# Attention, gated MLP and routed experts on one core: TensorE's operands moved to multiples of 512 bytes

## The reference, cut to what matters

```python
def reference(...):
    # 1. attention: B, H, S, D = 4, 8, 576, 64; each query sees itself and the 63 keys before it
    scores = np.matmul(q, k.transpose(0, 1, 3, 2)) / 8, masked to the window
    x = softmax(scores) @ v, laid out as 2304 tokens x 512
    # 2. gated MLP, d_ff = 1536
    xn = x / np.sqrt(np.mean(x * x) + 1e-06) * rms_g
    g, val = xn @ w_gate, xn @ w_val
    x = (g * sigmoid(g) * val) @ w_out
    # 3. 8 experts, top 2 of noisy logits per token
    noisy = x @ w_gate2 + log1p(exp(x @ w_noise)) * noise
    for e in range(8): out[mask] += weight * (np.maximum(x[mask] @ w1[e], 0) @ w2[e])   # 512 -> 1024 -> 512
```

## The kernel before, in words

| operand | offset | phase |
|---|---|---|
| `w_sb`, `ew_sb` (`W_OFF`) | 16512 | 128 |
| `ident`; `y_sb`, `yT_sb` | 180352; 172160, 166016 | 128 |
| `ones`, `tri`; `onesb` | 181376, 180864; 181120 | 128; 384 |
| `qbd`, `k_sb`, `v_sb`, `p_sb`, `pT_sb` | from 187616 | 224 |
| `mask_sb`, `identb` | 186336, 187360 | 480 |
| `xp`, `hp`, `sq` | 186336, 213984, 220128 | 480 |
| `x_row`, `xTh`, `xTl`, `relu`, `hTh`, `hTl` | from 194528 | 480 |

## Time and profile before

### The profile page before, as it was taken

The page is one execution under the profiler, slowest core; times in us unless marked ns, Lnnn a source line. Parts: engine busy times, 40 slices in busy tenths (PEclk is TensorE's granted clock), DMA queues, the critical chain, the costliest instruction groups (busy, mean ns, idle before and its releaser), DMA issues.

```text
span 1135.4 us, 20144 instructions
## 1 busy us (share of the span) xinstructions
PE 1112.4 (98%) x6285; PEld 961.4 (85%) x6286; DVE 540.7 (48%) x1166; ACT 324.2 (29%) x712; POOL 398.9 (35%) x370
## 2 busy tenths in 40 slices
PE   8999999999999999999999999999999999999996
PEld 7878999999998999999987888888888888888884
DVE  6776344353343443353456744445444544454442
ACT  7995122432331431432451020110202020200231
POOL 3567982022021120200386042240607060421485
PEclk9999999999999999999999999999999999999999
DMA  7975527013031030100356142241515151311565
GB/s 216 275 244 190 167 77 248 1 58 110 1 125 45 19 131 1 56 1 1 131 185 223 48 129 102 82 149 41 190 39 192 46 166 65 116 59 49 179 219 182
DMA packets 82732, 129.39 MB, mean 114 GB/s; under 512 B 6593, under 2 KB 38737, under 8 KB 82673
## 3 DMA queue, kind: packets, MB, share of 16 engines
q1 hardware_dynamic: 60816, 71.20, 19.4%
q10 hardware_dynamic: 16032, 38.47, 10.2%
q0 software_dynamic: 5824, 18.95, 5.1%
HBM read 85.87 MB, written 42.73 MB: 113 GB/s over the span
## 4 chain that ended last, share of the span: by engine, by line
PE 88%; POOL 4%; issue 3%; ACT 2%; DMA 2%; DVE 1%; POOLq 0%; ACTq 0%; DVEq 0%; SPq 0%
PE bank L774 26%; PE bank L965 18%; PE bank L937 18%; PE bank L806 13%; PE bank L978 3%; PE bank L720 3%; PE bank L747 2%; PE bank L949 1%; POOL token_rows_a L661 1%; PE bank L730 1%; PE bank L714 1%; DMA token_rows_b<-expert_rows,slots_u 1%; POOL expert_parts L645 1%; POOL token_rows_a L674 1%; PE bank L842 1%
## 5 line engine op out<-in xcount | busy, mean ns | idle before, releaser
L774 PE MATMUL bank<-x_parts,mlp_weights 128*128 128x384 f32 x1704 | 316.1, 341 | 0.0
L774 PEld LDWEIGHTS bank<-x_parts,mlp_weights 128*128 128x128 f32 x1704 | 300.6, 188 | 5.7 <-issue 0.3
L965 PE MATMUL bank<-expert_parts,hT_high 128*128 (+1 forms) x688 | 220.3, 401 | 1.4 <-DVE hT_low L1647 1.4
L937 PE MATMUL bank<-expert_parts,xT_high 128*128 (+1 forms) x688 | 220.3, 401 | 0.5 <-DVE xT_low L1636 0.5
L645 POOL TENSOR_TENSOR expert_parts<-raw_expert_a,expert_parts 128x512 fp32r<-128x512 f32 x64 | 81.5, 1311 | 266.7 <-ACT expert_parts L1249 266.7
L806 PE MATMUL bank<-mlp_weights,hidden_parts 128*128 128x512 f32 x648 | 163.9, 397 | 1.5 <-ACT y_sb L1173 1.5
L965 PEld LDWEIGHTS bank<-expert_parts,hT_high 128*128 128x128 f32 x688 | 126.3, 188 | 29.1 <-issue 1.7
L937 PEld LDWEIGHTS bank<-expert_parts,xT_high 128*128 128x128 f32 x688 | 126.2, 188 | 28.1 <-DVE xT_low L1636 0.8
L806 PEld LDWEIGHTS bank<-mlp_weights,hidden_parts 128*128 128x128 f32 x648 | 120.5, 188 | 26.2 <-ACT y_sb L1173 1.8
L965 PE MATMUL bank<-expert_parts,hT_low 128*128 (+1 forms) x344 | 136.1, 396 | 0.0
L937 PE MATMUL bank<-expert_parts,xT_low 128*128 (+1 forms) x344 | 136.0, 395 | 0.0
(11 more groups left out here) (205 smaller groups left out, 1244.6 us busy)
## 6 DMA issues: line engine op xcount, KB each, us to landing
raw_expert_a<-in_w ACTq DMA_DIRECT2D x32, 512.0 KB, 3.6
raw_expert_b<-in_w ACTq DMA_DIRECT2D x32, 512.0 KB, 4.0
x_row<-routed_rows SPq DMA_DIRECT2D x43, 256.0 KB, 2.7
expert_rows<-y_row SPq DMA_DIRECT2D x43, 256.0 KB, 2.0
expert_rows<-zeros SPq DMA_DIRECT2D x4, 2304.0 KB, 13.1
v_sb<-in_v SPq DMA_DIRECT2D x32, 256.0 KB, 3.7
q_sb<-in_qT SPq DMA_DIRECT2D x16, 288.0 KB, 3.7
k_sb<-in_kT SPq DMA_DIRECT2D x16, 288.0 KB, 4.2
```

The source lines that it names most:

```text
L774: last = nc.tensor.matmul(bank[:, 0:CHUNK], w_sb[:, i, wp, at:at + P], xp[:, par, part, k, :], start=n == 0, stop=n == 3 * KB - 1)
L937: last = nc.tensor.matmul(ps[half][:, 0:512], (xTh, xTl)[xp][:, k, :], ew_sb[:, bass.ds(slot, 1), wp, k * F2 + half * 512:k * F2 + half * ...
L965: last = nc.tensor.matmul(ps[5][:, 0:D], (hTh, hTl)[hp][:, f, :], ew_sb[:, bass.ds(slot, 1), 2 + wp, f * D:(f + 1) * D].rearrange("p a n - ...
```

## The change

It moves buffers and touches nothing else: every instruction, wait and transfer stays. `W_OFF` goes up by 384 bytes to 16896 (phase 0), and with it the staging area and `WORK_OFF`. `noise_sb`, `route_const` and `tri` leave `keep` for the free bytes behind `logitsT` in the staging area (offsets 179200 to 180608). `ones` now follows `ident` and `onesb` follows `ones`. `identb` moves from before `qbd` to behind `pT_sb` (220672), and `keep` is rounded up to a multiple of 512 (185344), where `att`, `mlp` and `moe` begin. By the code all operands of the table above then have phase 0 (`tri` 128; windows that step by 256 bytes have 0 or 256), and so have `raw_exp_a` and `raw_exp_b`. `rw_sb`, `lg_sb` and the small routing tables have other phases than 0 before and after.

```diff
--- before.py
+++ after.py
@@ -54,8 +54,10 @@
     xs_dram = nc.dram_tensor("routed_rows", [E * STRIDE, D], F32).ap()
     ye_dram = nc.dram_tensor("expert_rows", [ETILES * P, D], F32).ap()
 
+
+    ROW = 512
     base = 16512
-    W_OFF = base
+    W_OFF = (base + ROW - 1) // ROW * ROW
     STAGE_OFF = W_OFF + 6 * 6144 * 4
     WORK_OFF = STAGE_OFF + 4 * 4096
 
@@ -91,18 +93,22 @@
     assert D * 4 + CHUNK_TILES * KB * P * 4 <= 2 * 4096
     lgT_sb = at("logitsT", [P, P], F32, STAGE_OFF + 2 * 4096 + CHUNK_TILES * D * 4)
 
+
+    late = Area(STAGE_OFF + 2 * 4096 + CHUNK_TILES * D * 4 + P * 4)
+    noise_sb = late.take("noise_sb", [P, TILES, E], F32)
+    rc = late.take("route_const", [P, c_route.shape[1]], F32)
+    tri = late.take("tri", [P, P], BF16, 2)
+    assert late.pos <= WORK_OFF
+
     keep = Area(WORK_OFF)
     ident = keep.take("ident", [P, P], F32)
-    tri = keep.take("tri", [P, P], BF16, 2)
+    ones = keep.take("ones", [P, P], F32)
     onesb = keep.take("onesb", [P, P], BF16, 2)
-    ones = keep.take("ones", [P, P], F32)
     g_sb = keep.take("g_sb", [P, KB], F32)
 
     LOGITS = 32
     rw_sb = keep.take("rw_sb", [P, KB, LOGITS], F32)
-    noise_sb = keep.take("noise_sb", [P, TILES, E], F32)
     eps_sb = keep.take("eps_sb", [P, 2], F32)
-    rc = keep.take("route_const", [P, c_route.shape[1]], F32)
     slots_u = keep.take("slots_u", [P, TILES, 2], U32)
     slots_f = keep.take("slots_f", [P, TILES, 2], F32)
     top_all = keep.take("top_all", [P, TILES, 2], F32)
@@ -124,15 +130,16 @@
     slot_f = keep.take("slot_f", [P, CHUNK_TILES, 2], F32)
     slot_now = keep.take("slot_now", [P, CHUNK_TILES, 2], U32)
 
+    keep.pos = (keep.pos + ROW - 1) // ROW * ROW
     att = Area(keep.pos)
     mask_sb = att.take("mask_sb", [P, 4, P], BF16, 2)
-    identb = att.take("identb", [P, P], BF16, 2)
     qbd = att.take("qbd", [P, 2, NJ, P], F32)
     q_sb = att.take("q_sb", [P, 2, S], F32)
     k_sb = att.take("k_sb", [P, 2, S], F32)
     v_sb = att.take("v_sb", [P, 2, 2, 4, P], F32)
     p_sb = att.take("p_sb", [P, 3, GROUP, P], F32)
     pT_sb = att.take("pT_sb", [P, 2, GROUP, P], F32)
+    identb = att.take("identb", [P, P], BF16, 2)
     nb = att.take("nb", [P, 3, 4], F32)
     sm = att.take("sm", [P, 3, GROUP, 2], F32)
     rs = att.take("rs", [P, 3, 4], F32)
```

## The result

The changed kernel takes 1121.67 us (median of 4 runs, 1121.37 to 1124.06) where the kernel before took 1136.83 us (median of 4, 1136.42 to 1137.66): ratio 0.987, 95% interval 0.9853 to 0.9887. It is 15.2 us faster. The time lies inside the range given, near its lower end; "no change", the likeliest case, did not happen. How much of that is luck stands further down. The lines of the code are 7 higher than before: 774 is now 781, 806 is 813, 937 is 944, 965 is 972.

A forecast was written before the change was run, and what follows sets the result against it. TensorE's product count times pace was taken to bound the kernel up to 1113 us, then a tail. Products 0, other engines 0, transfers -0.3 us: 1137.2 - 0.3 = 1136.9 us, range 1118 to 1144 us.

The forecast's parts named there:

- no change: Whole kernel: time stays within about 0.2%, 2.3 us, likeliest between 1134.9 and 1139.5 us; chance 0.68.
- What bounds the kernel: Whole kernel: TensorE sets the end up to 1113 us, then a tail of gathers, sums and a store.
- The 85 us of unexplained time: MLP and expert products: 16.7 ns (384 columns) or 20.7 ns (512) each beyond one column per cycle, 85.0 us in all.
- That looks like a rate ..., which an offset doesn't change: Float32r products: four-byte columns arrive at a fixed rate, about 8 to 10% slow, so new starts gain 0 us.
- The ratio 1.24: Big products: excesses of 20.7 and 16.7 ns stand near 5 : 4, the 512-byte blocks touched, not 512 : 384.
- One block too many: Big products: uneven starts touch an extra 512-byte block; phase 0 saves 18.4 us, giving 1118.8 us; chance 0.10.
- The whole excess: Big products: all unexplained time comes from uneven starts, so 85.0 us go, giving 1052 us; chance 0.06.
- The two reads fall on the same place: Big products: moving and stationary operands at equal phases collide, 23.2 us slower, giving 1160 us; chance 0.14.
- Other engines at 0: DVE, ACT and POOL: moved tiles cost nothing; POOL's split of expert weights is covered by PE.
- Transfers at -0.3 us: Mask load, two gathers and last store on the chain: gain between 0 and 1.5 us, taken as 0.3.
- That PE would not wait more: PE: no instruction, wait or transfer is added or moved past another, so nothing queues behind anything new.
- The tail after the last product: End of the kernel: the tail gets shorter by no more than 1.5 us.

The follow-up runs named there:

- e3: The changed kernel with the weight area and the region behind `keep` both at phase 128: 1123.17 us, ratio 0.9868 to the kernel before.
- e4: The changed kernel with the weight area and the region behind `keep` both at phase 256: 1122.63 us, ratio 0.9863 to the kernel before.
- m1: The kernel before with only the weight area and the staging area behind it moved up by 352 bytes: 1125.07 us, ratio 0.9892.
- the control: The changed kernel itself, unchanged, run beside m1 on the same chip: 1122.25 us, ratio 0.9868 to the kernel before.

## Why the prediction was right and wrong

**What bounds the kernel** was right in the main: PE's pace times its 4440 float32r products, and a tail. But PE doesn't set the end up to 1113 us. Before, its last product starts at 1125.4 us, and the chain leaves it at 1067.9, so what nine of the 86 expert sets save is not on it. The 85 us of unexplained time were the right place to look; the change took 17.8 of them from the products.

**"That looks like a rate ..., which an offset doesn't change"** is the step that failed. I compared the moving operands' starts (480 and 128), then the stationary ones' (128 and 480), each by itself, and found no difference. From that I put the products at 0, and they gave 17.8 us. The runs showed that neither start matters and the distance between them does: 226.7 ns a product at distance 0, whatever the phase (0, 128, 256 or 480), where it was 234. Before the change the two distances were 352 and 160, modulo 256 96 and 160, and both stand at the slow end of the curve: 176.7, the slowest value measured for 384 columns, and 234. Two slow values looked like a law. The bf16 row that I set against them, `mask_sb` by `identb`, has distance 0 modulo 256 before and after, so it could show nothing of this and shows nothing on bf16. The ratio 1.24 that pointed to blocks was a coincidence of the same kind.

**The rivals.** "One block too many" gave 1118.8 us, 2.9 under what was measured, and is refuted as a cause by e3, e4 and m1. The whole excess did not go: 13.3 ns a product remain at the best distance found. "The two reads fall on the same place" named the right quantity and had its sign wrong: equal starts are the fast case. (I called both distances before 352; by the order of the operands they are 352 and 160.) What I held against it, the products of `qbd` and `k_sb`, had distance 0 modulo 256 for every window, so there was nothing to compare, and they were plain float32. On that type there is one row, the sums of squares: distance 352 before and 0 after, 485 and 484 ns.

**The range** holds the measured time by luck. Its lower end was put at 1118 us for the sake of "one block too many", whose mechanism the runs refute; the case that I gave 0.68 did not happen.

**Other engines at 0** was right: POOL's split takes 1301 and 1295 ns instead of 1311, beside PE. **Transfers at -0.3 us** were not resolved; the raw buffers, with no gain at phase 0, give no ground for them. That PE would not wait more was wrong by 2.6 us in the profiled execution, and by less in the control, where the wait for `so_far` is 0.7 us and there is none for `x_row`. The tail after the last product is not shorter either: its last start is 10.0 us before the end of the span, afterwards 11.4.

**The pace that the change could reach** is bounded by these rows: with 512 columns no series of float32r products settled below 226.7 ns at any of the 16 distances tried. The Trainium skill, page "TensorE: Matmul & The Clock Gate", section "Back-to-back issue gap", puts the warm gap at columns / 2.4 + 2.5 ns, an estimate of 215.8 for 512 columns; no run here agrees with it for float32r.

What stays open: why distance has this effect. That two reads of one product, or the stream and the next product's weight load, meet in the memory is the obvious thought, and it is only argued: narrower weights should then have helped. Width is the only thing of the load that was varied, so the thought isn't refuted either. Also open are the first three to ten steps of a set before it settles (behind transposes one of 314 to 321 ns, then others of 224 to 236), and what sets the length of that. At distance 0 they look like one fixed sequence that is entered at different points: 235, 233, 236, 224, 231, 236, 228, 232, 231 ns and then 227 in e3's sets down, the last eight of it in m1, the last two in the changed kernel's sets up. A set of nine products, as in the MLP down, ends before it settles: inside it the mean is 231.0 ns at distance 0, and at 64 it is 229.0.

## What to carry to other kernels

In a stage that is bound by float32r products, take the pace from starts in the trace and compare it with columns / 2.4 GHz. Then look at the start of the moving operand less that of the stationary one modulo 256 bytes: 0 is best for long sets of 512 columns (3% faster than 160, the slowest multiple of 32), 64 was better by 17 ns a set for the sets of nine, and 0, 64, 192 and 224 are about equal for 384. Place both operands by the same remainder; multiples of 512 do that, but so does any common one. And two slow cases that agree don't show that a quantity has no effect: ask what they have in common.

## What the runs showed that was not expected

The settled pace of float32r products depends on the two operands' distance, with a period of 256 bytes, and does so with every other engine idle. For 512 columns it is 226.7 ns at 0, 228.9 at 64, 232.6 to 234.3 at the other multiples of 32, and 236.7 at 4 bytes. At distance 0 the excess over the columns is the same 13.3 ns with 256, 384 and 512 columns (120.0, 173.3, 226.7 ns), 32 cycles of 2.4 GHz. A stationary operand of 32 columns instead of 128 makes the product slower, not faster (231.7 against 226.7 ns), though its load takes 109 ns and not 189.
